# Attention and expert kernel: the global queries' scores of all eight heads in one block of matmuls a batch

## The chip, the cores and the metric

The kernel runs on one core of a Trainium2 chip. The metric is the device time of one execution in microseconds (us). Engines: TensorE (PE, its weight loads PEld), VectorE (DVE), ScalarE (ACT), GpSimd (POOL); SyncE (SP) issues the transfers.

## The reference

Three stages, all in float32. An attention over 4 batches and 8 heads of width 64 with 512 local and 32 global tokens: global queries see all keys, local queries see the 32 global keys and the local keys within 32 positions. Then a soft mixture of 8 experts with 4 slots each, then a feed-forward layer of width 2048.

```python
k_all = np.concatenate([k_g, k_l], axis=2)
s_g = scale * np.matmul(q_g, k_all.transpose(0, 1, 3, 2))
out_g = np.matmul(sm(s_g), v_all)
s_ll = np.where(mask, scale * np.matmul(q_l, k_l.transpose(0, 1, 3, 2)), -1000000000.0)
s_l = np.concatenate([scale * np.matmul(q_l, k_g.transpose(0, 1, 3, 2)), s_ll], axis=-1)
out_l = np.matmul(sm(s_l), v_all)
...
h = g @ w_in
return ((h - np.tanh(h)) @ w_out).astype(np.float32)
```

## The kernel before, in words

Each engine has its own instruction list, and semaphores order them. The attention goes over 4 batches of U = 10 units: units 0 to 3 are local heads 0 to 3, unit 4 holds the global queries of heads 0 to 3 (quad 0), units 5 to 8 are local heads 4 to 7, unit 9 holds the global queries of heads 4 to 7 (quad 1). Heads come in pairs, since keys and queries lie with 64 dimensions of two heads on 128 partitions (`kT[0..3]`, `qT[0..3]`, and `qgT` for the global queries).

*TensorE* (`batch`, L609): in unit k it transposes the probabilities of unit k + 1 (`turn_probs`, L560 to L566, into banks 4 and 5, copied out by ScalarE, L930 and L932), then multiplies unit k's probabilities with the values (`weigh`, L581 for global units, L587 and L595 for heads). Some units end with a block of scores for five units ahead (`SCORES_AT`, L320): scores of a pair of heads at units 5, 7, 0 and 2 (L550: 16 matmuls on 64x64 places of the array), global scores at units 9 (for unit 4 of the next batch) and 4 (for unit 9). A global block (L541) has for each of four heads one matmul of 32 query columns against 512 keys and one against the 32 shared keys. A head has 64 rows and 32 columns of the array, so the four stand on four of eight such places: row half `j % 2`, column quarter `j`. Its results go to PSUM banks 0 and 1; the scores of even heads lie in banks 0 and 1 too, those of odd heads in banks 2 and 3. Before a block of scores TensorE waits until VectorE has taken the old scores from its banks (`masked_ready`); the wait (`wait_scores`, L517) stands ahead of the last four matmuls of `weigh`.

*VectorE* (`batch`, L1139): in unit k it normalises unit k's result (L1113 to L1123), then takes unit k + 5's scores from PSUM (`maxima`, L1086): for a head an addition of the mask (L1101, which sets `masked_ready`) and a maximum (L1106), for a global unit one reduction that copies and takes the maximum (L1092) and a small product (L1096). GpSimd subtracts the maximum (L457), ScalarE takes the exponential (L914, L922) two units ahead.

*SP* issues all loads in one order, each behind a semaphore wait (`keys`, `queries`, `global_queries`, `values`, L324 to L343): within a batch the keys and queries of the next one, one expert's first weights (`load_w1`, L312) and another's second (`load_w2`, L315), values, and the copies of the global rows (`spread_global`, L360). Ahead of the loop (L631 to L639) two blocks of head scores and one global block are made, with waits for the masks.

After the attention come the router, the experts (L746, L777), the product of their outputs with the first feed-forward weights in four parts (L875), and the feed-forward chunks (L821, L846, L849).

## Time and profile before

| | us |
|---|---|
| median of 3 runs | 318.64 (318.07 to 319.13) |
| profiled execution | 318.87 |
| its span | 317.1 |
| TensorE busy | 306.9 (97%) |
| VectorE busy | 211.9 (67%) |
| ScalarE busy | 139.0 (44%) |
| GpSimd busy | 64.8 (20%) |
| attention, global block ahead of the loop to the fourth batch's | 13.53 to 102.17 |

A busy TensorE counts overlapping matmuls with their pipeline's length, so the start of one group and the start of the next tell more than busy time. In the chain of waits TensorE has 86% of the span, VectorE 7%. A float32 matmul is two passes, and each is a record of its own: 8 matmuls are x16.

### The profile page before, as it was taken

To read this page: it belongs to the slowest core of one execution; us is meant where nothing else is said; L and a number is where in the kernel's file an instruction comes from. 1 tells how busy PE (TensorE), PEld (TensorE's weight loads), DVE (VectorE), ACT (ScalarE), POOL (GpSimd) and SP (SyncE) were. 2 spreads that over 40 slices of the span, in tenths; PEclk is the share of its full clock that TensorE was granted. 3 is DMA by queue.
4 is the path that set the end of the run, shared out by engine and by line. 5 is a ranking of instruction groups with operands and counts; after the bars stand their busy time and mean duration, and the time that the engine had idled before them with its cause. 6 is when DMAs were issued, how large, how long until landed. Compare 5 with 4: busy or idle time off the path is not lost.

```text
span 317.1 us, 7840 instructions
## 1 busy us (share of the span) xinstructions
PE 306.9 (97%) x2987; PEld 220.3 (69%) x2987; DVE 211.9 (67%) x443; ACT 139.0 (44%) x293; POOL 64.8 (20%) x62
## 2 busy tenths in 40 slices
PE   7999999999999999999998999999999999999994
PEld 4576777777777786233335888788888888888883
DVE  3887988888889556721258877566556666566572
ACT  1366766666566642111137554432334222532531
POOL 0543434434335001000008964000000000000000
PEclk9999999999999999999999999999999999999999
DMA  7999999999999969999999000030003000300202
GB/s 236 376 375 341 334 377 407 370 401 372 375 390 343 391 232 378 414 407 412 415 419 406 21 2 0 1 132 2 0 0 134 0 0 0 135 1 0 99 2 74
DMA packets 18032, 69.56 MB, mean 219 GB/s; under 512 B 4176, under 2 KB 5840, under 8 KB 14288
## 3 DMA queue, kind: packets, MB, share of 16 engines
q1 hardware_dynamic: 18000, 69.14, 57.7%
q8 instruction: 19, 0.31, 0.4%
q14 instruction: 13, 0.11, 0.1%
HBM read 64.41 MB, written 4.46 MB: 217 GB/s over the span
## 4 chain that ended last, share of the span: by engine, by line
PE 86%; DVE 7%; issue 5%; ACT 1%; POOL 1%; DVEq 0%; POOLq 0%
PE ps L846 20%; PE ps L849 20%; PE ps L550 6%; PE ps L595 5%; PE ps L821 5%; PE ps L746 4%; PE ps L777 4%; PE ps L587 3%; PE ps L566 3%; DVE sc L1101 3%; PE ps L606 2%; PE ps L541 2%; PE ps L560 2%; PE ps L581 2%; PE ps L658 1%
## 5 line engine op out<-in xcount | busy, mean ns | idle before, releaser
L849 PE MATMUL ps<-wlo,gg 128*128 128x512 f32 x204 | 80.5, 395 | 0.0
L846 PE MATMUL ps<-whi,gg 128*128 128x512 f32 x204 | 80.3, 394 | 0.0
L1307 DVE SCALAR_TENSOR_TENSOR nt<-uu,ps 128x512 f32<-128x512 f32 (+2 forms) x80 | 48.4, 607 | 47.3 <-ACT uu L1008 47.1
L1008 ACT ACTIVATE uu<-ps 128x512 f32<-128x512 f32 (+2 forms) x80 | 42.8, 537 | 84.0 <-PE ps L821 78.2
L457 POOL TENSOR_TENSOR sc<-sc,mx 128x640 f32<-128x640 f32 x32 | 40.1, 1253 | 53.5 <-DVE mx L1106 53.5
L1318 DVE TENSOR_TENSOR gg<-nt,ps 128x512 fp32r<-128x512 f32 (+2 forms) x80 | 47.9, 601 | 0.1
L846 PEld LDWEIGHTS ps<-whi,gg 128*128 128x128 f32 x204 | 38.4, 188 | 8.8
L849 PEld LDWEIGHTS ps<-wlo,gg 128*128 128x128 f32 x204 | 38.4, 188 | 8.0
L1101 DVE TENSOR_TENSOR sc<-ps,cst 128x640 f32<-128x640 f32 x32 | 26.2, 820 | 7.5 <-PE ps L550 5.9
L821 PE MATMUL ps<-cT,Pst 128*128 128x512 f32 (+2 forms) x80 | 28.9, 361 | 0.7 <-DVE Pst L1289 0.6
L595 PEld LDWEIGHTS ps<-vv,eT 128*64 128x64 f32 x512 | 18.7, 137 | 13.4 <-issue 11.0
L846 PE MATMUL ps<-whi_first,gg 128*128 128x512 f32 x68 | 26.9, 396 | 0.4 <-DVE gg L1318 0.4
L1106 DVE TENSOR_REDUCE mx<-sc 128x4 f32<-128x640 f32 x32 | 26.2, 820 | 1.1
L849 PE MATMUL ps<-wlo_first,gg 128*128 128x512 f32 x68 | 26.7, 392 | 0.0
L922 ACT ACTIVATE pr<-sc 128x512 f32<-128x512 f32 x32 | 20.2, 631 | 13.1 <-POOL sc L457 12.4
L595 PE MATMUL ps<-vv,eT 128*64 128x65 f32 x512 | 24.5, 230 | 1.2 <-DVE gmx L1092 0.3
L932 ACT COPY eT<-ps 128x512 f32<-128x512 f32 x40 | 23.5, 587 | 2.3
L930 ACT COPY eT<-ps 128x128 f32<-128x128 f32 (+1 forms) x40 | 10.5, 262 | 26.5 <-PE ps L564 14.7
L550 PE MATMUL ps<-kT,qT 64*64 64x160 f32 x512 | 21.1, 303 | 0.0
L587 PE MATMUL ps<-vg,eT 128*128 128x260 f32 x64 | 19.3, 383 | 0.0
L821 PEld LDWEIGHTS ps<-cT,Pst 128*128 128x128 f32 x80 | 15.1, 189 | 5.4 <-issue 2.0
L550 PEld LDWEIGHTS ps<-kT,qT 64*64 64x64 f32 x512 | 16.4, 133 | 1.1
(130 smaller groups left out, 384.6 us busy)
## 6 DMA issues: line engine op xcount, KB each, us to landing
w<-moe_w SPq DMA_DIRECT2D x11, 2048.0 KB, 11.2
vv<-v_t SPq DMA_DIRECT2D x8, 1170.0 KB, 7.7
w<-moe_w SPq DMA_DIRECT2D x14, 512.0 KB, 11.6
kT<-k_t SPq DMA_DIRECT2D x16, 416.0 KB, 6.3
out<-oo SPq DMA_DIRECT2D x17, 256.0 KB, 2.2
qT<-q_t SPq DMA_DIRECT2D x16, 256.0 KB, 7.3
win<-moe_w_in SPq DMA_DIRECT2D x4, 1024.0 KB, 16.6
wout<-moe_w_out SPq DMA_DIRECT2D x3, 1024.0 KB, 22.2
```

What stands on the lines that cost most here:

```text
L457: nc.gpsimd.tensor_tensor(by_j, by_j, m[:].unsqueeze(2).broadcast_to([P, 4, 160]), ALU.subtract).then_inc(lowered_ready, 1)
L550: mm = pe.matmul(o, qT[pr][r, 64 * t:64 * t + 64], seen_keys(pr, t)[r], start=True, stop=True)
L587: pe.matmul(cols(6 + k % 2, 4 * (D + 1)), et[:, 512:640], vg[qd][:, :, h, :], start=True, stop=False, skip_group_check=True)
L595: mm = pe.matmul(ps[64 * a:64 * a + 64, 6 + k % 2, (D + 1) * j:(D + 1) * (j + 1)], et[:, P * j + 64 * a:P * j + 64 * a + 64], v, start=Fal ...
L821: pe.matmul(cols(h_bank(i, c), width), Pst[:, P * c:P * c + P], c_cols(i, width), start=True, stop=True).then_inc(h_ready, 1)
L846: pe.matmul(o, g, hi, start=(c == 0), stop=False)
L849: mm = pe.matmul(o, g, lo, start=False, stop=(c == NC - 1))
L1008: nc.scalar.activation(uu[c % 2][:, 0:width], cols(h_bank(i, c), width), ACT.Square, scale=(1.0 / 3) ** 0.5).then_inc(square_ready, 1)
L1101: nc.vector.tensor_tensor(sc[h % 2][:].rearrange("p (b n) -> p b n", b=2), ps[:, bank:bank + 2, 0:320], cst[:, C_MASK:C_MASK + 640].rearra ...
L1106: nc.vector.tensor_reduce(mx[h % 2][:], sc[h % 2][:].rearrange("p (j n) -> p j n", j=4), AX.X, ALU.max).then_inc(max_ready, 1)
L1307: nc.vector.scalar_tensor_tensor(out=nt[c % 2][:, 0:width], in0=uu[c % 2][:, 0:width], scalar=1.0, in1=cols(h_bank(i, c), width), op0=ALU. ...
L1318: nc.vector.tensor_tensor(gg[c % 4][:, 0:width], nt[c % 2][:, 0:width], cols(h_bank(i, c), width), ALU.add).then_inc(g_ready, 1)
```

## The change

The global scores of all eight heads of a batch are made in one block, at unit 9 for the next batch. Quad 1 stands on the four places that quad 0 leaves free (`global_rows`: column quarter `j ^ qd`), and its scores go to banks 2 and 3. `SCORES_AT` loses the entry for unit 9. VectorE takes both quads' maxima one after the other at unit 9 (`global_maxima`), with a buffer and a maximum of its own for each quad; `rank` counts units in the order in which scores are now made (0 to 3, 4, 9, 5 to 8). SP loads keys of pairs 2 and 3 and the global queries of the next batch earlier. Lines of the changed kernel are 7 to 18 higher than before.

```diff
-        scg = place("scg", [P, SL + SG], F32)
+        scg = [place(f"scg{n}", [P, SL + SG], F32) for n in range(2)]
         mx = [place(f"mx{n}", [P, 4], F32) for n in range(2)]
-        gmx = place("gmx", [P, 2], F32)
+        gmx = [place(f"gmx{n}", [P, 2], F32) for n in range(2)]
...
-            return 0 if k in GQ else 2 * head_of(k)[1]
+            return 2 * (k // 5) if k in GQ else 2 * head_of(k)[1]
+
+        def rank(k):
+            return k if k < 5 else 5 if k == 9 else k + 1
+
+        def global_rows(qd, j):
+            return 32 * (j ^ qd)
 
         def unit_of(h):
             return h if h < 4 else h + 1
 
         def probs_of(k):
-            return scg if k in GQ else pr[k % 2]
+            return scg[k // 5] if k in GQ else pr[k % 2]
...
-        SCORES_AT = {(u - AHEAD) % U: u for u in (0, 2, 4, 5, 7, 9)}
+        SCORES_AT = {(u - AHEAD) % U: u for u in (0, 2, 4, 5, 7)}
...
-                sp.wait_ge(scores_ready, U * (i - 1) + GQ[pr // 2] + 1)
-                sp.dma_start(kT[pr][:], k_t[i - 1, pr]).then_inc(qk_loaded[pr], 16)
+                sp.wait_ge(scores_ready, U * (i - 1) + (6, 6, 8, 10)[pr])
+                sp.dma_start(kT[pr][:], k_t[i - 1, pr]).then_inc(qk_loaded[pr] if pr < 2 else global_loaded, 16)
 
             def queries(i, pr):
 
-                sp.wait_ge(scores_ready, U * (i - 1) + (2, 4, 7, 9)[pr])
-                sp.dma_start(qT[pr][:], q_t[i - 1, pr]).then_inc(qk_loaded[pr], 16)
+                sp.wait_ge(scores_ready, U * (i - 1) + (2, 4, 8, 10)[pr])
+                sp.dma_start(qT[pr][:], q_t[i - 1, pr]).then_inc(qk_loaded[pr] if pr < 2 else q_loaded[pr], 16)
 
             def global_queries(i):
-                sp.wait_ge(scores_ready, U * i)
-                sp.dma_start(qgT[:], qg_t[i - 1]).then_inc(qg_loaded, 16)
+                sp.wait_ge(scores_ready, U * (i - 1) + 6)
+                sp.dma_start(qgT[:], qg_t[i - 1]).then_inc(global_loaded, 16)
...
             global_queries(1)
+            keys(1, 2)
+            keys(1, 3)
             sp.wait_ge(zeros_ready, 2)
             values(1, 0)
-            keys(1, 2)
             queries(1, 2)
-            keys(1, 3)
             queries(1, 3)
             values(1, 1)
...
                 keys(i + 1, 1)
                 queries(i + 1, 0)
                 queries(i + 1, 1)
+                global_queries(i + 1)
+                keys(i + 1, 2)
+                queries(i + 1, 2)
                 load_w1(sp, i - 1, w1_loaded, w1s[i - 1][:])
-                keys(i + 1, 2)
                 keys(i + 1, 3)
-                global_queries(i + 1)
+                queries(i + 1, 3)
                 values(i + 1, 0)
-                queries(i + 1, 2)
-                queries(i + 1, 3)
                 spread_global(i, 0)
...
-                    pe.wait_ge(qg_loaded, 16 * i)
-                    pe.wait_ge(masked_ready, U * i + k - 1)
+                    pe.wait_ge(global_loaded, 48 * i)
                 else:
-                    pe.wait_ge(qk_loaded[head_of(k)[0]], 32 * i)
-                    pe.wait_ge(masked_ready, U * i + k)
+                    pair = head_of(k)[0]
+                    pe.wait_ge(*((qk_loaded[pair], 32 * i) if pair < 2 else (q_loaded[pair], 16 * i)))
+                pe.wait_ge(masked_ready, U * i + rank(k))
...
-                    for part in range(2):
+                    def one(qd, j, part):
+                        pr = 2 * qd + j // 2
+                        r = slice(64 * (j % 2), 64 * (j % 2) + 64)
+                        own = kT[pr][r, 0:768].rearrange("r (b n) -> r b n", n=96)[:, :, 0:64]
+                        keys = kT[pr][r, 768:768 + SG] if part else own
+                        at = global_rows(qd, j)
+                        o = ps[at:at + 32, scores_ps(GQ[qd]) + part, 0:SG if part else 512]
+                        return pe.matmul(o, qgT[r, pr, :], keys, start=True, stop=True)
+
+                    for j in range(4):
+                        for qd in range(2):
+                            one(qd, j, 0)
+                    for qd in range(2):
                         for j in range(4):
-                            pr = 2 * (k // 5) + j // 2
-                            r = slice(64 * (j % 2), 64 * (j % 2) + 64)
-                            own = kT[pr][r, 0:768].rearrange("r (b n) -> r b n", n=96)[:, :, 0:64]
-                            keys = kT[pr][r, 768:768 + SG] if part else own
-                            o = ps[32 * j:32 * j + 32, bank + part, 0:SG if part else 512]
-                            mm = pe.matmul(o, qgT[r, pr, :], keys, start=True, stop=True)
-                    mm.then_inc(scores_ready, 1)
+                            mm = one(qd, j, 1)
+                        mm.then_inc(scores_ready, 1)
...
+            def global_maxima(i):
+                for qd in range(2):
+                    k = GQ[qd]
+                    dve.wait_ge(scores_ready, U * i + rank(k) + 1)
+                    dve.wait_ge(probsT_ready, U * (i - 1) + k + 1)
                     dve.sem_inc(passed_by_dve, 1)
                     nc.vector.tensor_tensor_reduce(
-                        scg[:], cols(scores_ps(k), SL + SG), cst[:, C_ZERO:C_ZERO + 1].broadcast_to([P, SL + SG]),
-                        1.0, -3.0e38, ALU.add, ALU.max, gmx[:, 0:1]).then_inc(masked_ready, 1)
-                    dve.wait_ge(masked_ready, U * i + k + 1)
-                    nc.vector.tensor_scalar(gmx[:, 1:2], gmx[:, 0:1], -SCALE, None, ALU.mult).then_inc(gmax_ready, 1)
-                else:
-
-                    dve.wait_ge(exp_ready, U * i + (unit_of(h - 2) if h >= 2 else unit_of(h + 6) - U) + 1)
-                    bank = scores_ps(k)
-                    nc.vector.tensor_tensor(sc[h % 2][:].rearrange("p (b n) -> p b n", b=2),
-                                            ps[:, bank:bank + 2, 0:320],
-                                            cst[:, C_MASK:C_MASK + 640].rearrange("p (b n) -> p b n", b=2),
-                                            ALU.add).then_inc(masked_ready, 1)
-                    dve.wait_ge(masked_ready, U * i + k + 1)
-                    nc.vector.tensor_reduce(mx[h % 2][:], sc[h % 2][:].rearrange("p (j n) -> p j n", j=4),
-                                            AX.X, ALU.max).then_inc(max_ready, 1)
+                        scg[qd][:], cols(scores_ps(k), SL + SG), cst[:, C_ZERO:C_ZERO + 1].broadcast_to([P, SL + SG]),
+                        1.0, -3.0e38, ALU.add, ALU.max, gmx[qd][:, 0:1]).then_inc(masked_ready, 1)
+                for qd in range(2):
+                    dve.wait_ge(masked_ready, U * i + rank(GQ[qd]) + 1)
+                    nc.vector.tensor_scalar(gmx[qd][:, 1:2], gmx[qd][:, 0:1], -SCALE, None, ALU.mult).then_inc(gmax_ready, 1)
...
-                    if k + 5 < U:
+                    if k + 5 < U - 1:
                         maxima(i, k + 5)
-                    elif not last:
+                    elif k == U - 1 and not last:
+                        global_maxima(i + 1)
+                    elif k + 5 >= U and not last:
                         maxima(i + 1, k + 5 - U)
...
-            for k in range(5):
-                if k == GQ[0]:
-                    dve.wait_ge(const_loaded, 16)
+            for k in range(4):
                 maxima(1, k)
+            dve.wait_ge(const_loaded, 16)
+            global_maxima(1)
             with dve.Fori(1, NB) as i:
```

TensorE at unit 9, before (end of the unit and the block; `kT_55` to `kT_58` are the keys of pairs 0 to 3, `vv_66` the values of quad 1):

```order
L581 MATMUL ps<-vv_66,eT_73 32x65 x4
L541 MATMUL ps<-kT_55,qgT 32x512 x2
L541 MATMUL ps<-kT_56,qgT 32x512 x2
L541 MATMUL ps<-kT_55,qgT 32x32 x2
L541 MATMUL ps<-kT_56,qgT 32x32 x2
L640 REGISTER_ALU
L640 COMPARE_AND_BRANCH
```

and now:

```order
L594 MATMUL ps<-vv_66,eT_73 32x65 x4
L547 MATMUL ps<-kT_55,qgT 32x512
L547 MATMUL ps<-kT_57,qgT 32x512
L547 MATMUL ps<-kT_55,qgT 32x512
L547 MATMUL ps<-kT_57,qgT 32x512
L547 MATMUL ps<-kT_56,qgT 32x512
L547 MATMUL ps<-kT_58,qgT 32x512
L547 MATMUL ps<-kT_56,qgT 32x512
L547 MATMUL ps<-kT_58,qgT 32x512
L547 MATMUL ps<-kT_55,qgT 32x32 x2
L547 MATMUL ps<-kT_56,qgT 32x32 x2
L547 MATMUL ps<-kT_57,qgT 32x32 x2
```

The block of pairs 2 and 3, which stood at unit 4, has joined the block at unit 9; at unit 4 no scores follow the weighted sums.

VectorE at unit 9, now (before, one reduction and one product stood between the normalisation, which ends with `xg_53`, and the branch):

```order
L1122 TENSOR_REDUCE mx_77<-sc_69 128x4
L1129 TENSOR_SCALAR den<-ps 128x1
L1131 RECIPROCAL rden<-den 128x1
L1136 TENSOR_SCALAR xg_53<-ps,rden 128x64
L1102 REGISTER_ALU
L1105 ISA scg_74,gmx_78<-ps,cst 128x544
L1105 ISA gmx_78 128x1
L1102 REGISTER_ALU
L1105 ISA scg_75,gmx_79<-ps,cst 128x544
L1105 ISA gmx_79 128x1
L1110 TENSOR_SCALAR gmx_78<-gmx_78 128x1
L1110 TENSOR_SCALAR gmx_79<-gmx_79 128x1
```

The second reduction (`scg_75`) came from unit 4, where VectorE now only normalises.

SP within a batch, now (`w_0_113` is a first weight, `vv_64` the values of quad 0):

```order
L343 DMA qgT<-qg_t 128x128
L334 DMA kT_57<-k_t 128x832
L339 DMA qT_61<-q_t 128x512
L319 DMA w_0_113<-moe_w 128x4096
L334 DMA kT_58<-k_t 128x832
L339 DMA qT_62<-q_t 128x512
L348 DMA vv_64<-v_t 128x2340
L350 DMA vg_65<-vg_t 32x260 x4
L372 DMA x<-xg_52 32x64 x4
```

Before, the weight stood ahead of both keys, the global queries behind them, and the queries of pairs 2 and 3 behind the values.

## Rows read from the trace of the kernel before

**Rows 1.** The page, section 2: mean busy share of the 16 DMA engines, in tenths, 40 slices.
```profile
DMA  7999999999999969999999000030003000300202
```
**Rows 2.** Timeline of the weight loads (PEld), around 166 us: start us, us, engine line op out<-in xcount [idle before <-releaser].
```profile
166.63 0.16 PEld L875 LDWEIGHTS ps<-win,soT 128*32 128x32 f32 x8 [0.36 <-DMA win<-moe_w_in]
```
**Rows 3.** Two stretches (busy by engine, PEclk, DMA share, GB/s) and SP's timeline.
```profile
114.00:116.00 2.00, 2.00 (x41) 1.80 (x33) 0.95 (x3) 0.58 (x1) 0.00 (x0) 1.00 0.35 96
116.00:118.00 2.00, 2.00 (x43) 1.64 (x41) 1.47 (x3) 0.59 (x1) 0.00 (x0) 1.00 0.44 91
...
115.08 1.68 SPq L312 DMA_DIRECT2D w<-moe_w  x1
```
**Rows 4.** Timeline of the weight loads in one block of global scores, unit 4.
```profile
51.22 0.15 PEld L541 LDWEIGHTS ps<-kT,qgT 64*32 64x32 f32 x8
51.67 0.13 PEld L541 LDWEIGHTS ps<-kT,qgT 64*32 64x32 f32 x4 [0.30 <-issue]
52.10 0.13 PEld L541 LDWEIGHTS ps<-kT,qgT 64*32 64x32 f32 x4 [0.30 <-issue]
```
**Rows 5.** Timeline of the matmuls behind that block: unit 5 and its scores.
```profile
52.27 0.33 PE L560 MATMUL ps<-cst,pr 128*128 128x128 f32 x1
...
54.21 1.32 PE L550 MATMUL ps<-kT,qT 64*64 64x160 f32 x32
55.46 0.33 PE L560 MATMUL ps<-cst,pr 128*128 128x128 f32 x1
```
**Rows 6.** Timeline ahead of the loop, 12 to 15 us, TensorE and VectorE.
```profile
12.25 0.83 DVE L1101 TENSOR_TENSOR sc<-ps,cst 128x640 f32<-128x640 f32 x1 [1.33 <-ACT pr L923]
...
12.50 0.49 PE L566 MATMUL ps<-cst,pr 128*128 128x128 f32 x3
...
13.53 1.12 PE L541 MATMUL ps<-kT,qgT 64*32 64x512 f32 x16
13.85 0.82 DVE L1101 TENSOR_TENSOR sc<-ps,cst 128x640 f32<-128x640 f32 x1
...
14.59 0.33 PE L560 MATMUL ps<-cst,pr 128*128 128x128 f32 x1
```
**Rows 7.** Timeline of units 8 and 9 of the second batch, TensorE and VectorE.
```profile
60.57 0.33 PE L560 MATMUL ps<-cst,scg 128*128 128x128 f32 x1
...
62.32 0.33 PE L560 MATMUL ps<-cst,pr 128*128 128x128 f32 x1
...
63.30 0.81 DVE L1101 TENSOR_TENSOR sc<-ps,cst 128x640 f32<-128x640 f32 x1
63.73 1.12 PE L541 MATMUL ps<-kT,qgT 64*32 64x512 f32 x16
...
65.56 0.72 DVE L1092 CUSTOM_DVE_ANT_0 scg<-ps,cst 128x544 f32<-128x544 f32 x1
...
66.33 0.15 DVE L1096 TENSOR_SCALAR gmx<-gmx 128x1 f32<-128x1 f32 x1
```
**Rows 8.** Timeline of units 6 and 7 of the first batch: a full wait for a mask.
```profile
30.55 0.33 PE L560 MATMUL ps<-cst,pr 128*128 128x128 f32 x1
...
34.14 0.20 PEld L595 LDWEIGHTS ps<-vv,eT 128*64 128x64 f32 x4 [0.28 <-DVE sc L1101]
34.41 1.32 PE L550 MATMUL ps<-kT,qT 64*64 64x160 f32 x32
```
**Rows 9.** Timeline of the matmuls: what follows three batches' last blocks and the fourth's only one.
```profile
39.88 0.33 PE L560 MATMUL ps<-cst,pr 128*128 128x128 f32 x1
...
64.79 0.33 PE L560 MATMUL ps<-cst,pr 128*128 128x128 f32 x1
...
89.70 0.33 PE L560 MATMUL ps<-cst,pr 128*128 128x128 f32 x1
...
102.17 0.33 PE L560 MATMUL ps<-cst,pr 128*128 128x128 f32 x1
```
**Rows 10.** The page, section 6: loads of the values, KB each, median us from issue to landing.
```profile
vv<-v_t SPq DMA_DIRECT2D x8, 1170.0 KB, 7.7
```

29 lines of the change are left out of this document (18 added, 11 removed).

## The prediction, on record before the changed kernel ran

> **What bounds the kernel now.** Three views, in this order. The page's DMA line [rows 1] shows the transfer engines full from the second to the 22nd of its 40 slices but for one. The list of TensorE's waits holds almost nothing in the attention stage, yet one row later is telling: at 166.63 the fourth part of the expert-to-output product waits 0.36 us for its transfer [rows 2]. So two things run side by side up to there, the chain of matmuls and the stream of loads, and a gain of the first reaches the end only if the stream comes forward too. The stretches around 116 us [rows 3] show that it can: between the last weights issued during the attention and the next ones the share of DMA is 0.35 and 0.44, which is (0.65 + 0.56) x 2 = 2.4 us of nothing to carry, and what ends this is the load issued at 115.08 [rows 3], which stands in SP's queue behind the copies of the last batch's global rows, so behind the end of the attention. **If the attention ends up to 2.4 us sooner, matmuls and loads both move by all of it.** After 180 us TensorE works without a wait and DMA idles.
>
> So the change is worth what it saves between the start and the end of the attention. There TensorE is the chain, but VectorE is close behind: the timeline shows which waits end last.
>
> **What the change removes.** A block of global scores takes from 51.22 [rows 4] to 52.27 [rows 5] = 1.05 us. In it the weights of four small matmuls, both passes of each, are loaded at once; the next loads come 0.45 and 0.43 us later, when the second pass and the products with the 32 shared keys start [rows 4]. So four places of the array work side by side, pass after pass, and 0.17 us are left for the shared keys. Eight such blocks run now: one ahead of the loop, one at unit 4 of all four batches, one at unit 9 of three.
>
> **What it adds.** Four blocks with eight matmuls of 512 columns at once. I take the two passes as they are and add the issue of twice as many instructions: 16 more small passes and four more large ones at an estimated 5 ns each (the loads of eight passes lie within 0.15 us, and most of that is the length of one), in round numbers 0.1 us, of which I take 0.08: **1.13 us a block**. The bounds: 1.05 (nothing added) and 0.45 + 3 x 0.43 + 2 x 0.17 = 2.1 us (two rows of places after one another). I take the low end because score matmuls on 64x64 places already use both row halves over the same columns at once, into different banks, and 16 of them, 32 passes, take 1.25 us (54.21 to 55.46 [rows 5]): eight rounds of four, 0.16 each, about what 160 columns need at the rate of 512 in 0.43.
>
> **The Trainium skill speaks against this.** The row first: in [rows 4] matmuls on row half 0 and on row half 1 write bank 0 together, on different partitions, and start together. "TensorEngine Tiling (Array Packing)", section Restrictions and Gotchas, says that different row tiles cannot access the same PSUM bank simultaneously. By it the halves would take turns, as the upper bound has it; the trace disagrees already for the block of before.
>
> **What it moves: waits.** This is where most of the gain goes. Units are numbered by k; a unit's scores are computed five units ahead.
>
> (a) *Ahead of the loop.* The block needed the mask addition of head 2 (12.25 + 0.83 = 13.08) and started 0.45 us after it, at 13.53; now it uses all four banks and needs that of head 3, 13.85 + 0.82 = 14.67 [rows 6]. New start 15.12, new end 16.25 instead of 14.59: **+1.66 us**. Keys of pairs 2 and 3 are then there: they are issued ahead of the values now, behind the global queries.
>
> (b) *Unit 9.* The block waits for the mask of head 3 of the next batch instead of head 2. Count from the end of the scores before it, 60.57 [rows 7]: the mask of head 3 is done at 63.30 + 0.81 = 64.11, the block started at 63.73. A wait releases the unit's last small matmuls 0.05 us after the addition, and the next block follows 0.27 us behind (34.14, 34.41 [rows 8]). So it starts at 64.43, or 3.86 us after the scores, where it was 3.16: **+0.70 us** in each of three batches. It is no accident of lateness: the head pairs show the same chain, 30.55 to 34.41 = 3.86 [rows 8] (two units of matmuls, a normalisation and a mask between two sets of scores).
>
> (c) *Unit 0.* The scores of head 4 go into banks 0 to 3, so both maxima of global scores must be through. One reduction starts 0.77 us before its small successor (65.56, 66.33 [rows 7]), and 0.73 us after its start it is done. VectorE will stand ready when the block ends, since TensorE waited in (b); an estimate from these: start 0.15 us behind the block, second one 0.77 later, done 0.73 later, release at 1.71. Without a wait a unit lets its scores start after 1.75 us (60.57 to 62.32), its last matmuls at 1.48: stall 0.23 us.
>
> (d) *Units 4 and 5.* Nothing global any more: 62.32 to 63.73 = 1.41 us for unit 4 [rows 7]. Unit 5 took 52.27 to 54.21 = 1.94 us [rows 5], 0.19 of it waiting for the global maximum; now 1.75. The next stall, if one comes, is ScalarE's copying, which for one unit needs more than these 1.41 us; up to 0.1 us in the last batch.
>
> **The sum.** From the end of a block to the end of the next, after the change: unit 0 and scores 1.98 + 1.25; units 1, 2 and scores 3.86 + 1.25; units 3, 4 1.75 + 1.41; unit 5 and scores 1.75 + 1.25; units 6, 7 and scores 3.86 + 1.25; units 8, 9 3.86; block 1.13: 24.60 us. Before [rows 6, 9]: 39.88 - 14.59 = 25.29, then 24.91 twice. Differences -0.69, -0.31, -0.31. The fourth batch runs from the block to the end of unit 4 in 3.23 + 5.11 + 3.16 = 11.50 us, before 102.17 - 89.70 = 12.47 [rows 9]: -0.97; with (d) -0.87. Together 1.66 - 0.69 - 0.31 - 0.31 - 0.87 = **-0.5 us**. Four saved blocks are 4.2 us of matmuls; 3.7 of them are given back.
>
> Loads that are moved: w1 comes behind the global queries and one pair more, the values of quad 0 behind w1 and all queries. The queue's order changes, its bytes don't. The values land 7.7 us after their issue in the median [rows 10], and they stand to lose most: two loads of queries come before them now, 0.5 MB, some 1.3 us at the page's 370 to 400 GB/s. Issued once unit 4 has used the old ones, 11.5 us after a block, they land some 9 to 11.5 us later at worst, and are needed 1.1 us behind the next block, 25.7 us after this one. I cost it at nothing; if that cover goes, units wait for keys at unit 9 or for values at unit 0.
>
> The profiled execution took 318.87 us, 0.23 over the median of 318.64. It would become 318.4; the median **318.1**. A measurement of this kernel can tell 0.3%, 0.96 us, from no change: 317.7 to 319.6 counts as the same.
>
> **The rivals.**
>
> *A, slower: the eight places don't work at once.* Each block takes 2.1 us; 4 x 0.97 = 3.9 more, 322.0 us. For it: no row has more than four places in flight, and the bank rule above. Against it: all four-place rows run at full rate, in both shapes. It decides from (0.5 + 0.96) / 4 = 0.37 us over 1.13, a block of 1.5 us. Chance 0.12.
>
> *B, faster: the new wait of (b) isn't paid.* VectorE loses a global unit at unit 4 and could run ahead, so that the masks of heads 2 and 3 come 0.7 us sooner: 3 x 0.70 = 2.1, 316.0 us. It is bounded by the gap of 2.4 us in the loads. Against it: the chain of (b) starts at scores that TensorE itself produces after that, so a lead is lost again. A part of it, or a shorter start in (a), is easily possible. Chance 0.14.
>
> *C, the same, but for another reason:* the attention ends sooner, and the loads don't, because the weights issued before 103 us fill the gap. Then the part at 166.63 waits for its transfer and everything ends at 318.6. Chance 0.08.
>
> *D, slower: TensorE's clock.* It idles from 12.99 to 14.8 us now (its last transposes start at 12.50, 0.49 [rows 6]). The granted clock is 1.00 (2.4 GHz) in the rows read [rows 3], and none shows a fall or such a gap. Should it go to 1.2 GHz there for, say, 4 us (an assumption), half of these are lost, 2 us: 320.1. Chance 0.06.
>
> **How the numbers follow.** The forecast has 0.60; its own range is 317.4 to 318.9 (mask waits and blocks 0.1 to 0.2 us off, four times), wholly within the bound but for its low end. Faster: 0.12 of it and B's 0.14, 0.26. Same: the other 0.48 and C's 0.08, 0.56. Slower: A and D, 0.18. The range 316.9 to 320.4 takes in the forecast, C, D and the weak half of B; A and the strong half of B, 0.19, lie outside.
>
> **What would show it.** The block: 16 large passes in two groups 0.45 us apart, its end 1.13 us from its start; A shows four groups. The block ahead of the loop at 15.1, ending at 16.2 us. At unit 9 the second half of the weighted sums waits for "sc L..." of VectorE, 0.7 us; unit 5 waits no more. Period 24.6 us. The end of unit 4 of the fourth batch at 101.5 us. The load of 115.08 at 114.5, and the wait of 166.63 kept, half a microsecond sooner. The step I trust least is (b) with (c), a chain over two engines put together from rows that show it elsewhere. I would be wrong if the period came out under 24.3 or over 24.9 us, or if a load's landing released a matmul before 110 us.

## The result: 0.3% slower, and the profile after

The changed kernel takes **320.06 us** (median of 21 executions, 319.05 to 324.67), the kernel before in the same session 319.12 (21, 318.07 to 320.27); the execution of 324.67 us is disturbed and left out of the comparison. Ratio **1.0026**, 95% interval 1.0016 to 1.0037. So it is slower by 0.9 us, inside the bound of 0.3% but on the wrong side: the forecast was 0.5 us faster. The profiled execution took 319.95 us with a span of 318.2 (before: 318.87 and 317.1), the mean granted clock is 0.999.

TensorE's waits first. Timeline of the changed kernel ahead of the loop (start us, us, engine line op out<-in xcount [idle before <-releaser]); these rows answer to [rows 6].

```profile
12.44 0.49 PE L579 MATMUL ps<-cst,pr 128*128 128x128 f32 x3
...
13.88 0.81 DVE L1117 TENSOR_TENSOR sc<-ps,cst 128x640 f32<-128x640 f32 x1
...
14.84 0.38 PE L519 MATMUL ps<-cst 128*128 128x32 f32 x2 [1.91 <-DVE sc L1117]
15.15 0.66 PE L547 MATMUL ps<-kT,qgT 64*32 64x512 f32 x8
```

The block starts at 15.15 where 15.12 was forecast: it waits for VectorE's mask of head 3, which ends at 14.69, and follows 0.46 us later. The same view at unit 9 of the first batch and the block behind it, which makes the scores of the second, answering to [rows 7]:

```profile
38.44 0.67 PE L594 MATMUL ps<-vv,eT 128*32 128x65 f32 x32
39.59 0.32 PE L594 MATMUL ps<-vv,eT 128*32 128x65 f32 x8 [0.48 <-DVE sc L1117]
39.84 1.15 PE L547 MATMUL ps<-kT,qgT 64*32 64x512 f32 x32
40.92 0.33 PE L573 MATMUL ps<-cst,pr 128*128 128x128 f32 x1
```

From 39.84 to 40.92 the block of all eight heads takes 1.08 us. Its weight loads, answering to [rows 4], show that all eight places work together: sixteen (eight matmuls, two passes) are issued within 0.18 us, the next eight follow 0.45 us later and the next 0.43 us behind those.

```profile
39.84 0.18 PEld L547 LDWEIGHTS ps<-kT,qgT 64*32 64x32 f32 x16
40.29 0.15 PEld L547 LDWEIGHTS ps<-kT,qgT 64*32 64x32 f32 x8 [0.28 <-issue]
40.72 0.15 PEld L547 LDWEIGHTS ps<-kT,qgT 64*32 64x32 f32 x8 [0.27 <-issue]
```

Blocks start at 15.15, 39.84, 64.57 and 89.31, so a batch takes 24.69, 24.73 and 24.74 us (24.60 forecast). The last batch is where the order fails to pay. Timeline of all engines of the changed kernel, from unit 4 on:

```profile
100.65 0.33 PE L573 MATMUL ps<-cst,pr 128*128 128x128 f32 x1
...
101.45 0.59 ACT L945 COPY eT<-ps 128x512 f32<-128x512 f32 x1
101.52 0.81 DVE L1117 TENSOR_TENSOR sc<-ps,cst 128x640 f32<-128x640 f32 x1
...
102.19 0.30 PE L573 MATMUL ps<-cst,pr 128*128 128x128 f32 x1
...
103.27 1.25 POOL L464 TENSOR_TENSOR sc<-sc,mx 128x640 f32<-128x640 f32 x1 [1.24 <-DVE mx L1122]
...
104.55 0.63 ACT L935 ACTIVATE pr<-sc 128x512 f32<-128x512 f32 x1 [1.01 <-POOL sc L464]
...
105.43 0.59 ACT L945 COPY eT<-ps 128x512 f32<-128x512 f32 x1
...
106.17 0.30 PE L573 MATMUL ps<-cst,pr 128*128 128x128 f32 x1 [0.43 <-ACT eT L945]
...
109.64 0.55 PE L619 MATMUL ps<-cst,x 128*128 128x128 f32 x3
```

Unit 4 ends at 102.19, 0.02 us behind the 102.17 of [rows 9]; it took 1.54 us, since ScalarE's copy of 101.45 ends at 102.04 and the transposes of 102.19 follow 0.15 us behind it. Then unit 8's mask (101.52), GpSimd's subtraction (103.27) and ScalarE's exp (104.55) come one after another, ScalarE's copy of unit 7's probabilities (105.43) stands behind that exp in its queue, and TensorE idles 0.43 us in unit 7, ahead of the transposes of unit 8's probabilities, which again follow 0.15 us behind the end of that copy. The profiles of e5, e9 and e12 below have the same wait of 0.43. In the kernel before, the rows of the same view show no wait:

```profile
104.39 0.27 ACT L930 COPY eT<-ps 128x128 f32<-128x128 f32 x1
104.72 0.58 ACT L932 COPY eT<-ps 128x512 f32<-128x512 f32 x1
...
105.67 0.33 PE L560 MATMUL ps<-cst,pr 128*128 128x128 f32 x1
...
109.18 1.09 PE L606 MATMUL ps<-cst,x 128*128 128x128 f32 x8
```

The attention part, counted to the first matmul that turns the tokens, ends at 109.64 instead of 109.18: **0.46 us later, not 0.5 sooner**. From there 52.25 us of work are the same in both kernels (161.89 and 161.44 for the end of the experts' layers). Then the loads matter once more. PEld in the product of [rows 2], changed kernel:

```profile
165.67 0.16 PEld L888 LDWEIGHTS ps<-win,soT 128*32 128x32 f32 x8 [0.94 <-DMA win<-moe_w_in]
168.19 0.16 PEld L888 LDWEIGHTS ps<-win,soT 128*32 128x32 f32 x8 [1.22 <-DMA win<-moe_w_in]
```

From the end of the experts' layers to the first product of the feed-forward part it takes 172.00 - 161.89 = 10.11 us here and 9.50 before: another 0.61. And the stretch that ended with the load of 115.08 [rows 3], now of 115.55, carries less:

```profile
112.00:114.00 2.00, 2.00 (x40) 1.89 (x28) 1.57 (x5) 0.77 (x2) 0.00 (x0) 1.00 0.41 152
114.00:116.00 2.00, 2.00 (x43) 1.66 (x41) 1.06 (x3) 0.55 (x2) 0.00 (x0) 1.00 0.15 39
116.00:118.00 2.00, 2.00 (x43) 1.70 (x41) 1.38 (x2) 1.02 (x2) 0.00 (x0) 1.00 0.55 111
```

The DMA share is 0.41, 0.15 and 0.55, (0.59 + 0.85 + 0.45) x 2 = 3.8 us of nothing to carry (before 0.93, 0.35, 0.44: 2.6). So the transfer engines had more time to spare there, not less; whether the 0.61 belongs to the change is for a second profile.

### The profile page after: what moved, and what is told of

Its sections match the earlier page's. It is cut to its first block, busy times and chain, and to the rows that moved or that the text cites. A ratio compares the mean times of both kernels' runs of the same rounds, so it can differ in the third digit from the quotient of the medians.

```text
span 318.2 us, 7836 instructions
## 1 busy us (share of the span) xinstructions
PE 304.1 (96%) x2987; PEld 218.6 (69%) x2987; DVE 211.0 (66%) x443; ACT 137.8 (43%) x293; POOL 64.8 (20%) x62
## 4 chain that ended last, share of the span: by engine, by line
PE 78%; DVE 9%; DMA 7%; issue 3%; ACT 1%; POOL 1%; SPq 0%; DVEq 0%
PE ps L859 20%; PE ps L862 20%; DMA win<-moe_w_in 7%; PE ps L563 6%; PE ps L834 5%; PE ps L608 4%; PE ps L759 4%; DVE sc L1117 4%; PE ps L619 2%; PE ps L600 2%; PE ps L579 2%; PE ps L514 2%; PE ps L573 2%; PE ps L547 2%; PE ps L671 1%
```

## The experiments

T1 is the theory that the order of the work decides: the matmul time saved went into waits for VectorE and ScalarE. T2 is that the reordered loads decide. T3 comes with e9, T4 with e11, T5 with e13. "A batch" is the time between starts of global blocks in the profile, second to third and third to fourth batch where they differ; "end" is the first matmul that turns the tokens, in the same profile; ratios are to the kernel before, run beside. Between sessions the median of the kernel before lay at 318.83 to 319.36, so medians of different sessions compare to some 0.3 us at best.

| run | median us | ratio, 95% | a batch, us | end, us |
|---|---|---|---|---|
| changed kernel | 320.06 | 1.0026 (1.0016 to 1.0037) | 24.74 | 109.64 |
| e1 four places | 323.30 | 1.0137 (1.0103 to 1.0170) | 25.58 | 112.97 |
| e2 weights first | 320.33 | 1.0036 (1.0020 to 1.0052) | 24.74 | 109.95 |
| e3 four swaps | 321.04 | 1.0064 (1.0044 to 1.0085) | 25.09 | 111.18 |
| e4 four swaps, on before | 318.34 | 0.9976 (0.9959 to 0.9992) | 24.89 | 108.65 |
| e5 changed kernel again | 320.05 | 1.0030 (1.0014 to 1.0045) | 24.74 | 110.90 |
| e6 kernel before again | 318.72 | 0.9993 (0.9981 to 1.0006) | 24.91 | 108.73 |
| e7 cover back | 321.12 | 1.0066 (1.0041 to 1.0091) | 24.74, 25.23 | 111.74 |
| e8 last batch, swap at 3 | 320.81 | 1.0076 (1.0046 to 1.0106) | 24.75 | 110.90 |
| e9 swap at 8 | 320.18 | 1.0023 (1.0005 to 1.0041) | 24.77 | 110.19 |
| e10 swap at 1 | 318.74 | 0.9982 (0.9968 to 0.9996) | 24.38 | 108.50 |
| e11 clock kept | 319.62 | 1.0015 (0.9999 to 1.0031) | 24.73 | 109.32 |
| e12 swaps at 1, 6, clock kept | 318.39 | 0.9987 (0.9966 to 1.0009) | 24.06 | 108.97 |
| e13 values earlier | 320.02 | 1.0015 (0.9989 to 1.0042) | 24.74 | 109.59 |
| e14 e12 and e13 together | 317.97 | 0.9962 (0.9935 to 0.9988) | 24.06, 24.44 | 108.08 |
| e15 swaps at 1, 6, on before | 317.73 | 0.9946 (0.9922 to 0.9970) | 24.28 | 107.70 |
| e16 e15, weights behind values | 327.46 | 1.0232 (1.0185 to 1.0279) | late loads | 118.41 |
| e17 e15, weights behind queries | 325.95 | 1.0187 (1.0144 to 1.0230) | late loads | 116.89 |

**e1, four places.** Heads j and j+4 write the same rows, so four places of the array serve eight heads; the output is the same.

```diff
-            return 32 * (j ^ qd)
+            return 32 * j
...
-                                           et[:, P * c + 32 * j:P * c + 32 * j + 32], ve[qd][:, j ^ qd, c, :],
+                                           et[:, P * c + 32 * j:P * c + 32 * j + 32], ve[qd][:, j, c, :],
```

> Change kept whole, but heads j and j+4 write to the same rows (32*j), so that a block has four places of the array instead of eight; all waits and loads stay as they are. T1 (what the change saved is the block's own time, and new waits gave it back): the block ahead of the loop takes 1.9 to 2.1 us instead of 1.08, unit 9 to 10 of three batches each 0.9 longer, every block is on the path, the attention part ends 3.5 to 4 us later, and the time is 3 to 4 us above the changed kernel (about 323.5). T2 (the later end comes from the reordered loads, and PE's order in the attention part hardly counts): attention part later as above, but the product part still waits for the same weight loads, so under 2 us of it shows at the end.

The block's weight loads of the large matmuls now come in four groups, 40.64, 41.10, 41.53 and 41.96, and the block takes 40.64 to 42.64 = 2.00 us. The end is 3.33 us later, the time 3.24 us higher. T1 holds, T2 (under 2 us) doesn't: what TensorE gains or loses in a block is passed on nearly whole, 0.92 a block as measured, 0.84 a batch.

**e2, weights first.** One line of SyncE's queue put back.

```diff
                 queries(i + 1, 1)
+                load_w1(sp, i - 1, w1_loaded, w1s[i - 1][:])
                 global_queries(i + 1)
                 keys(i + 1, 2)
                 queries(i + 1, 2)
-                load_w1(sp, i - 1, w1_loaded, w1s[i - 1][:])
```

> Change kept, but the expert weight load goes back to where it stood on SyncE's queue: right behind queries 1, ahead of the global queries and of keys and queries 2. T1: nothing is late for want of a load in the attention part, time the same as the changed kernel within 0.3 us; the first wait for a block stays that for VectorE's mask. T2 (the reordered loads made it slower): the time falls by 0.5 us or more, to that of the kernel before or below it. A third outcome: keys 2 and 3 now land behind 2 MB of weights and the block waits for them, 1 us or more slower.

No difference that the intervals can tell. T1, as far as the place of this load goes.

**e3 and e4, four swaps.** VectorE masks and reduces the scores of unit k+5 before it normalises unit k; e3 on the changed kernel, e4 on the one before.

```diff
-                    normalise(i, k)
+                    swap = k in (1, 3, 6, 8) and not (last and k >= 5)
+                    if not swap:
+                        normalise(i, k)
...
+                    if swap:
+                        normalise(i, k)
```

> Change kept, but at units 1, 3, 6 and 8 VectorE masks the scores of unit k+5 before it normalises unit k (not in the last batch's second half). T1: the 0.70 us stall at unit 9 and those of about 0.3 us ahead of the pairs of scores go, a unit batch takes 23.3 to 24.0 us instead of 24.7, the attention part ends 3 to 5 us sooner; of that 2 us or more is seen at the end of the kernel. T2: the attention part ends sooner, but the weight loads of the product part don't come sooner by as much, and the time stays within 1 us of the changed kernel.

> The same swap on VectorE in the kernel before (blocks of one quad of heads each, two a batch). T1: here too the stalls ahead of pairs of scores go, but with the waits gone PE's own work counts, and the changed kernel has 1 us a batch less of it: with the swap the changed kernel is ahead of this one by 2.5 us or more. T2: the two with the swap are within 1 us of each other, since neither is bound by PE's work of the attention part.

Both expectations fell: with the swaps the changed kernel got slower, a batch of 25.09 us, and the kernel before faster. TensorE's rows of e3 in the third batch:

```profile
68.52 0.34 PE L608 MATMUL ps<-vv,eT 128*64 128x65 f32 x4 [0.60 <-DVE gmx L1105]
...
79.59 0.71 PE L600 MATMUL ps<-vg,eT 128*128 128x260 f32 x2 [0.78 <-DVE x L1139]
```

The wait for masks at unit 2 is gone, but new ones stand at units 0 and 5: for the two global maxima, which come behind the normalising of unit 8 now, and for a unit that VectorE normalises late. VectorE is busy 20.93 of the 25.09 us of that batch; moving work forward on it moves other work back.

**e5 and e6, both kernels again.** No edit.

> The changed kernel as it is, profiled a second time. In its first profile the attention part ended 0.46 us later than in the kernel before, and TensorE then waited 0.6 us longer for the weights of the product part (from the end of the expert layers, 161.89, to the first product of the feed-forward part, 172.00: 10.11 us, against 9.50 in the kernel before and in the three experiments so far). T1 (the attention part alone is later): this stretch is 9.50 again, attention end 109.6 to 110.0, the sum of both near +0.5 to +0.9 against before. T2 (the loads in their new order leave the weights late): 10.0 or more again.

> The kernel before as it is, profiled a second time, to learn how much the starts of its stages vary: expected the first block of global scores within 0.4 us of 13.54, attention end within 0.4 us of 109.18, and 9.50 us from the end of the expert layers to the first product of the feed-forward part. Ratio of its time to the runs of before 1.000 within 0.001.

e5: from the experts' layers to the first product 172.66 - 163.16 = 9.50 us. So the 0.61 us of the first profile isn't of the change; e6, the kernel before, has 9.65. e6 starts its first block at 13.08 and ends at 108.73, 0.45 us sooner each than the first profile of the same kernel and just outside the 0.4 that was expected: one profile's start or end is known no better than that. What lies between repeats: from the start of the first block to the end it is 95.65 us in both profiles of the kernel before, and in the changed kernel's 109.64 - 15.15 = 94.49 us, with 94.49, 94.49 and 94.52 in e2, e11 and e13. So the change saves 95.65 - 94.49 = 1.16 us there, and the later start, 1.62 us, turns this into a loss.

e5's end of 110.90 lies 0.9 us over the expectation. The first batch took 41.08 - 15.04 = 26.04 us, and three stretches of it tell why (the third number from the end is the granted clock):

```profile
14.00:16.00 2.00, 1.27 (x18) 0.74 (x26) 1.40 (x2) 0.78 (x2) 1.67 (x2) 0.85 1.11 379
16.00:18.00 2.00, 2.00 (x30) 1.52 (x15) 1.01 (x3) 0.31 (x2) 0.77 (x1) 0.50 0.98 406
18.00:20.00 2.00, 2.00 (x35) 1.27 (x37) 0.89 (x6) 1.32 (x3) 0.00 (x0) 0.79 1.11 254
```

And from its timeline:

```profile
14.73 0.38 PE L519 MATMUL ps<-cst 128*128 128x32 f32 x2 [1.82 <-DVE sc L1117]
15.04 1.78 PE L547 MATMUL ps<-kT,qgT 64*32 64x512 f32 x32
```

The granted clock fell to 0.50, 1.2 GHz, right behind the wait of 1.82 us ahead of the first block, and the block took 1.71 us. Among this kernel's 31 executions eleven have a mean clock of 0.995 or less; among the 22 of the kernel before that ran beside e5 none is under 0.998. That is rival D. e8's profile shows it too (0.52 from 16.00 to 18.00, first batch 25.97 us), the other eight profiles with this wait don't. The mean of 0.994 in e5's profile is what such a stretch leaves; in the executions without a profile the mean alone is known, not where the clock was low. Its price in the median is small: of the thirty executions compared, the twenty at full clock have a median of 319.96, the ten others 320.12, far less apart than the 1.35 us that e5's profile lost in its first batch.

**e7, the cover back.** Behind unit 4 of the last batch TensorE does matmuls of the size of the block that the change took away there; the result is unused.

```diff
+                    if last and k == 4:
+                        pe.wait_ge(masked_ready, U * NB + rank(7) + 1)
+                        for part in range(2):
+                            for j in range(4):
+                                r = slice(64 * (j % 2), 64 * (j % 2) + 64)
+                                pe.matmul(ps[32 * j:32 * j + 32, part, 0:32 if part else 512], cst[r, 0:32],
+                                          cst[r, 0:32 if part else 512], start=True, stop=True)
```

> Changed kernel plus work of the size of the block that the change took out of the last batch: behind unit 4 of the last batch, eight matmuls of the same shapes on four places (two of 512 columns a place in turn, then the small ones), on the table of constants, into banks that are free then; the result isn't used. T1 (in the last batch the block covered the chain mask, maximum, GpSimd's subtraction, ScalarE's exp, so that without it 0.5 us of its 1.05 come back as a wait at unit 6): the wait of about 0.5 us ahead of unit 7 goes, the attention part ends 0.4 to 0.6 us later than in the changed kernel. Rival (the wait there has nothing to do with the block): it ends 1.0 to 1.1 us later and the wait stays.

```profile
100.50 0.33 PE L573 MATMUL ps<-cst,scg 128*128 128x128 f32 x1
...
103.67 1.12 PE L648 MATMUL ps<-cst 64*32 64x512 f32 x16
...
108.23 0.33 PE L573 MATMUL ps<-cst,pr 128*128 128x128 f32 x1
...
111.74 0.44 PE L619 MATMUL ps<-cst,x 128*128 128x128 f32 x2
```

Nothing waits at 108.23 any more, where the transposes of unit 8 begin. From unit 4's transposes to the end it is 111.74 - 100.50 = 11.24 us, in the changed kernel 109.64 - 98.90 = 10.74: 1.05 us of work cost 0.50. **The block in the last batch was worth only half its length; the other half covered the chain over VectorE, GpSimd and ScalarE.** The median is 1.07 us over e5's beside it, and the end 2.10 us over the first profile's. So the median doesn't decide between T1 and its rival; the stretch behind unit 4 does. The profile shows what else is later, ahead of the inserted work, where nothing was edited: the third batch took 25.23 us, with 0.3 us of waiting for queries, and the fourth begins with this:

```profile
92.94 0.68 PE L600 MATMUL ps<-vg,eT 128*128 128x260 f32 x2 [1.41 <-issue]
```

The last of the values of this batch landed at 92.85 in this execution, by the landings in the trace. In the changed kernel's first profile they landed at 90.36 and were used at 90.99. They are the longest under way of their kind there, 11.2 us; the row on the small loads of values of the changed kernel (line 350; the large ones of the kernel before had a median of 7.7 [rows 10]). In the first profile of the kernel before the same values landed at 89.63, 0.67 us ahead of their use at 90.30, so this cover was thin before the change too:

```profile
DMA to landing us min/median/max: 5.0/7.9/11.2
```

**e8, the same chain sooner.** The swap only at unit 3 of the last batch (swap = last and k == 3).

> Changed kernel, only that in the last batch at unit 3 VectorE masks and reduces unit 8's scores before it normalises unit 3. T1: mask 8 starts when its buffer is free (ScalarE's exp, about 101.0) instead of 101.52, the chain behind it comes 0.4 to 0.5 us sooner, the wait ahead of unit 7 falls from 0.43 to under 0.1, the attention part ends 0.3 to 0.5 us sooner. Rival (unit 5's weighing then waits for VectorE's late normalising of unit 3, as in the run with four swaps): no gain, or up to 0.5 us later.

The wait ahead of unit 8 is gone, and a wait of 0.67 us for the late normalising of unit 3 stands at unit 5: from the last block to the end 110.90 - 90.10 = 20.80 us, changed kernel 109.64 - 89.31 = 20.33. The rival holds.

**e9, the wait of step (b) alone.** swap = k == 8 and not last.

> Changed kernel, with the mask of head 3 of the next batch (which the block waits for at unit 9, 0.7 us) taken ahead of normalising unit 8, and nothing else moved. T1 (TensorE's own work and one late mask decide): the block starts 0.6 us sooner in each batch, a batch takes 24.1 us instead of 24.74, three times 0.6 at the end. T3 (new, after the four swaps: from the first mask of the next batch to the two maxima of the block VectorE has nearly no idle time, 0.4 of 9.9 us, so its work sets when the next scores may start, and the order within it doesn't count): the block starts 0.6 us sooner, the wait behind it, ahead of the scores of unit 5, grows from 0.33 to about 0.9, and a batch takes 24.6 to 24.8 us.

```profile
64.56 1.15 PE L547 MATMUL ps<-kT,qgT 64*32 64x512 f32 x32
...
67.98 0.34 PE L608 MATMUL ps<-vv,eT 128*64 128x65 f32 x4 [0.60 <-DVE gmx L1105]
```

T3: the 0.7 us ahead of the block are gone and the wait behind it has grown by 0.54 us (the next scores start 68.25 - 64.56 = 3.69 us after the block's start instead of 67.72 - 64.57 = 3.15). A batch takes 24.76 and 24.77 us. So the late mask of head 3 is only where the price shows; T3 puts it down to VectorE's chain of work around the block, which this outcome fits and e12 limits.

**e10, the swap at unit 1** (swap = k == 1).

> Changed kernel, with the swap at unit 1 alone (mask and maximum of unit 6 ahead of normalising unit 1), in all four batches. Here VectorE still waits 0.4 us for the scores of the next batch's unit 0, so what TensorE gains in the first half of a batch comes through. T1 and T3 alike: the wait of 0.35 us ahead of the scores of unit 7 goes, nothing takes its place (unit 3's weighing, which waits for unit 1 to be normalised, stands behind 1.3 us of scores), a batch takes 24.3 to 24.5 us instead of 24.74 and the attention part is over 1.2 to 1.5 us sooner. If a weighing waits instead, 24.7 or more.

A batch takes 24.38 us twice, and from the last block to the end it is 19.99 instead of 20.33: as expected. The time of 318.74 is the first of a variant of the changed kernel below the kernel before (e4's 318.34 was a variant of that one).

**e11, the clock kept.** One line, ahead of the wait for the first block.

```diff
             turn_probs(1, 0)
+            stay_awake(3, 6, cst)
```

> Changed kernel plus three matmuls of 128x512 on the table of constants in the wait of 1.9 us ahead of the first block; results unused. In the second profile of the changed kernel TensorE's granted clock was 0.85, 0.50 and 0.79 in the three stretches of 2 us from 14.00 on (1.2 GHz at the lowest), and the first batch took 26.04 us instead of 24.69; 11 of the changed kernel's 31 executions show a mean clock of 0.995 or less, none of the kernel before does. T4 (the new wait ahead of the first block lets the clock fall in some executions): with the wait filled no execution has a mean clock of 0.995 or less, the first batch takes 24.7, and the median falls by 0.1 to 0.4 us. Rival (the clock has another cause): a third of the executions show it as before.

All 12 executions have a mean clock of 0.997 or more, and the first batch takes 24.70 us. With e12 and e14, which have the same three matmuls, it is none of 30 executions at 0.995 or less; of the changed kernel and its eight variants without them (e1 to e3, e7 to e10, e13) it is 34 of 103. So T4 stands for the clock. The median is 0.44 us lower than the first of the changed kernel, but the intervals of the ratios overlap, so a gain isn't shown. The three matmuls also have a price: the block now starts behind them, 0.88 us after the end of head 3's mask (13.95 to 14.83) instead of 0.46. The same in e14:

```profile
12.76 2.74 PE L514 MATMUL ps<-cst 128*128 128x512 f32 x6
...
13.87 0.81 DVE L1118 TENSOR_TENSOR sc<-ps,cst 128x640 f32<-128x640 f32 x1
...
15.57 1.15 PE L547 MATMUL ps<-kT,qgT 64*32 64x512 f32 x32
```

Two matmuls instead of three might have kept the clock without it; no run tried that. "TensorE: Matmul & The Clock Gate" of the Trainium skill, Part 1, has idle TensorE fall to half its clock; the trace agrees, and shows that the same program's gap of 1.8 to 1.9 us does it in one execution and not in the next.

**e12, swaps at 1 and 6, clock kept** (swap = k == 1 or k == 6 and not last).

> Changed kernel with the swaps at units 1 and 6 (6 not in the last batch) and the three matmuls ahead of the first block. T3: the swap at unit 6 adds nothing to that at unit 1, since VectorE works without a gap from there on: a batch takes 24.3 to 24.5 us, the time is that of the run with the swap at unit 1 less 0.1 to 0.4 us, about 318.3. T1: the swap at unit 6 gives another 0.35 us a batch, 24.0 us, and about 317.3 in all.

A batch takes 24.06 us: T1 was right and T3 wrong on unit 6, whose swap gives another 0.32. So the order within VectorE's chain does count at some places. But the last batch lost it again:

```profile
91.00 0.68 PE L600 MATMUL ps<-vg,eT 128*128 128x260 f32 x2 [1.22 <-issue]
```

The values landed at 90.91. In this profile the stream of loads is the next bound, with TensorE some 1.4 us sooner at the last block than in the changed kernel.

**e13 and e14, values earlier**, on the changed kernel and on e12.

```diff
-                load_w1(sp, i - 1, w1_loaded, w1s[i - 1][:])
                 keys(i + 1, 3)
                 queries(i + 1, 3)
                 values(i + 1, 0)
+                load_w1(sp, i - 1, w1_loaded, w1s[i - 1][:])
```

> Changed kernel, with the first expert layer's 2 MB put behind keys 3, queries 3 and values 0 on SyncE's queue instead of ahead of them. In the changed kernel the last values 0 land at 90.36, 0.63 us ahead of their first use at 90.99. T5 (the values at the end of the reordered loads are late in a part of the executions): they now land before 87, slack over 3 us; the period stays 24.74, the median falls by 0.1 to 0.3 us. T1 (order of the work alone): they land sooner and the median stays within 0.1 us of 320.06. If moving the weights back costs: 0.3 us or more slower.

> The run with the swaps at units 1 and 6 and three matmuls ahead of the first block, plus the order of loads of the run before. There a batch took 24.06 us, but in the last batch TensorE waited 1.22 us for the values (landed 90.91, used at 91.00). T5: this wait goes, the attention part ends about 1.2 us sooner (107.8 for a first block at 15.8), the time is 317.0 to 317.6, clearly below the kernel before. Rival (the loads as a whole are the bound there, and something else of them is late next): 318.1 or more.

e13: the values land at 86.85, 4.1 us ahead of their use, and the median is 320.02, that of the changed kernel. Beside it the kernel before had 319.36, and with six executions the interval of the ratio, 0.9989 to 1.0042, takes in both no difference and the 0.9 us. So nothing here shows a part of the loads in the 0.9 us, and a small one isn't excluded. e14: from the last block to the end 20.00 instead of 21.04 us, so T5 names e12's wait rightly; 317.97 is 1.4 us under the kernel before beside it (319.36), though it misses the expectation by 0.4. In its third batch TensorE waited for queries (0.2 us), and that batch took 24.44 us.

**e15, e16, e17: the same edits on the kernel before.** e15 takes e12's swaps. e16 puts the weights behind values 0, e17 behind queries 3 as well (the diff is e13's in the other order of that kernel).

> The kernel before with the swaps at units 1 and 6 (6 not in the last batch). Its two blocks of four heads stand at units 9 and 4. T: the waits ahead of the pairs of scores go here too, 0.3 us each, but the values of the last batch then come only 0.1 us before their use, as with the four swaps; about 318.0.

> The same with the first expert layer's 2 MB behind keys 2, keys 3, the global queries and values 0. If the block of eight is worth its 1 us a batch less of TensorE's work once the waits are out: this kernel 0.5 us or more above the changed kernel with the same edits. If the mask of head 3 at unit 9 and ahead of the loop gives it all back: within 0.3 us of it or below.

> The kernel before with the swaps at units 1 and 6 and the first expert layer's 2 MB behind keys 2 and 3, the global queries, values 0 and queries 2 and 3. If the values held it: the wait of 1.0 us in the last batch goes, a batch stays 24.3 us, time 316.7 to 317.3. If the queries, now ahead of the weights but asked for late, or the idle stretch before the weights make something else late: 317.7 or more.

e15 is the fastest of all, 317.73, and isn't told apart from e14's 317.97. From the first block to the fourth it takes 86.42 - 13.27 = 73.15 us there and 88.08 - 15.57 = 72.51 in e14, from the fourth to the end 21.28 and 20.00; but the first block starts 2.30 us later in e14. So in these two profiles the block of eight saves 0.64 us in three batches and 1.28 in the last, 1.00 of it a wait that e15 alone has, and the late start costs more than both. But 0.42 us of that start are of the three unused matmuls, as e11 showed; the 1.88 left are about what the block saves. No run has e14 without them, so which kernel is the better base for the swaps stays open. That wait is for values that land at 89.15, though the profile's row names another releaser:

```profile
89.24 0.68 PE L587 MATMUL ps<-vg,eT 128*128 128x260 f32 x2 [1.00 <-DVE xg L1120]
```

e16 and e17 were to cure that and came out 8 to 10 us over e15; neither outcome that e16 was given fits. The mean clock is 0.982 and 0.984 in their profiles, so part of this is TensorE's clock behind its new waits. TensorE's waits in e16 (us in total, times, longest), and SyncE's queue in e17:

```profile
PE ps L595 <- DMA qT<-q_t: 6.3, 3, 2.8
```
```profile
75.64 0.43 SPq L332 DMA_DIRECT2D qT<-q_t  x1
82.17 0.81 SPq L327 DMA_DIRECT2D kT<-k_t  x2
```

In e16 queries wait behind 2 MB of weights. In e17 nothing is issued from 76.1 to 82.2 us, since the kernel before may load keys 2 only after its second block, and the weights that used to fill this wait stood behind it. The changed kernel asks for them at 72.24, and e13 shows no cost of the same move there.

## Why the prediction was wrong

**Right.** The block: 1.08 us measured, 1.13 forecast, eight places at once; rival A fell at 1.08, and e1 shows the 2.0 us of it. (a): start 15.15 and end 16.23, forecast 15.12 and 16.25. (b): the last matmuls of unit 9 wait for the mask of head 3, and the block starts 3.85 us after the scores (85.46 to 89.31), forecast 3.86. The cover of the moved loads held in the profile, with 0.63 us left; e7, e9, e10 and e12 show how thin it is.

**Wrong, in sizes, most of it in step (d).** By its own sum the prediction has unit 4 of the fourth batch end at 16.25 + 3 x 24.60 + 11.60 = 101.65 (its list of signs says 101.5), and nothing lost behind it. Measured are 102.19 and 0.44 us more behind it, 0.98 us off together:
- *Three periods*, "24.60 us": 24.69 to 24.74, so that the fourth block ends at 90.39 instead of 90.05: 0.34 us. Unit 4 takes 1.54 us in every batch and not the 1.41 of step (d), since TensorE waits for ScalarE's copying (0.39 in three batches). Unit 0 takes 2.02, 2.07 and 2.07 us instead of step (c)'s 1.98 (0.22). The shorter block and small differences give 0.27 back.
- *Fourth batch to the end of unit 4*, 11.60 with (d)'s 0.1: 102.19 - 90.39 = 11.80, 0.2 us. The scores of unit 5 start 2.16 us behind the block instead of 1.98 (step (c)).
- *Last batch behind unit 4*, costed at nothing: 109.64 - 102.19 = 7.45 against 109.18 - 102.17 = 7.01 before, 0.44 us. This is the largest single term.

**The step that failed** is (d): "The next stall, if one comes, is ScalarE's copying ... up to 0.1 us in the last batch". The runs show 0.13 us in each of four batches and 0.43 in unit 7 of the last, 0.95 where 0.1 was counted. I counted ScalarE's copying for one unit, and not what stands ahead of it in its queue: in the last batch the exp of unit 8, which waits for a chain of mask, maximum and subtraction that starts 3.0 us earlier on another engine. e7 shows this part by experiment: with the block's time back, the wait of 0.43 is gone. The 0.13 a batch and (c)'s excess are read from rows, and no experiment takes them out.

The 0.98 us turn 0.5 sooner into 0.46 later, the measured end. The chance of 0.18 for slower stood on rivals A and D, neither of which made this difference. Rival B had it the other way: e9 removed the wait of (b), and nothing was won. Rival C didn't arise, since the attention part ended no sooner.

**What the 0.46 doesn't cover.** The medians differ by 0.94. The first block starts at 15.15 in one profile and 13.53 in the other, 1.62 apart where 1.59 was forecast; over the ten profiles that share the changed kernel's start it lies at 14.64 to 15.60 with mean 15.20, over six with the start of the kernel before at 13.08 to 14.04 with mean 13.50: 1.70 apart, 0.1 more. The clock (rival D, given 0.06) adds about 0.1 to the median. Some 0.3 us stay without a name, less than the start of the first block varies from one execution to the next. The late start is the largest price of the change, and no experiment removes it: a block of four heads ahead of the loop with the block of eight inside it wasn't tried.

## What to carry to other kernels

Matmul time that another engine's chain runs beside isn't saved by removing it: before costing a removed block, follow every queue that ran under it to its next release, with what stands ahead in that queue. Where two engines are both nearly full (here TensorE 96% and VectorE 86% of a batch), moving one wait often moves it elsewhere. The two moves that paid, at units 1 and 6, delayed work that had 1.3 us of scores to cover it; at unit 3 the changed kernel has no scores behind unit 4 for that, and at unit 8 the move only passed the wait on to the two global maxima. When a reordering of loads looks free, look at the landing nearest to its use in several executions, not in one.

## What the hardware showed that I had not expected

Eight matmuls on 64x32 places, two row halves by four column quarters, ran at once, each at the rate of the block of four, with both halves writing the same two PSUM banks on different partitions: 512 columns in 0.45 and 0.43 us, 1.08 us a block for eight heads where four heads took 1.05. "TensorEngine Tiling (Array Packing)" of the Trainium skill, Restrictions and Gotchas, says that different row tiles can't access one bank simultaneously; the measurement decides against it for fp32 matmuls that write different partitions of the bank.

Behind a gap of 1.8 to 1.9 us of TensorE the granted clock fell to half in two of the ten profiles that have this gap (0.50 in e5, which has another gap of 0.77 us ahead of it, and 0.52 over a stretch in e8, which has not) and stayed at 1.00 in the rest. 34 of 103 executions with the gap have a mean clock of 0.995 or less, and none of 30 whose gap holds three unused matmuls.
